# FFT and two-layer MLP kernel: half of the turns as quarter products, filters in places of their own, second slot's first product ahead of V's second half

## The reference, cut to what matters

```python
def _attn_ref(x, filt_r, filt_i):            # x: (2, 3008, 256)
    X = np.fft.rfft(x, axis=1)
    F = (filt_r + 1j * filt_i)[None, :, :]
    y = np.fft.irfft(X * F, n=x.shape[1], axis=1)
    return y.astype(np.float32)

def _moe_ref(x, w_in, w_out):                # (6016, 256) x (256, 2048) x (2048, 256)
    h = x @ w_in
    g = np.maximum(0.01 * h, h)
    return (g @ w_out).astype(np.float32)

def _moe2_ref(x, w_in, w_out):               # the same with g = relu(h) ** 2
    ...

def reference(**kwargs):
    x = _attn_ref(...).reshape(B * S, D)
    return _moe2_ref(_moe_ref(x, ...), ...)
```

## Time and profile before

| | us |
|---|---|
| median of 3 runs | 1065.01 |
| the profiled execution, its own time | 1064.64 |
| its span in the trace | 1062.5 |
| TensorE busy | 1057.0 (99% of the span) |
| VectorE (DVE) busy | 827.9 (78%) |
| ScalarE (ACT) busy | 563.3 (53%) |
| GpSimd (POOL) busy | 316.1 (30%) |

### The profile page before, as it was taken

The page is one execution under the profiler, slowest core; times in us unless marked ns, Lnnn a source line. Parts: engine busy times, 40 slices in busy tenths (PEclk is TensorE's granted clock), DMA queues, the critical chain, the costliest instruction groups (busy, mean ns, idle before and its releaser), DMA issues.

```text
span 1062.5 us, 13988 instructions
## 1 busy us (share of the span) xinstructions
PE 1057.0 (99%) x5120; PEld 879.8 (83%) x5120; DVE 827.9 (78%) x1142; ACT 563.3 (53%) x979; POOL 316.1 (30%) x287
## 2 busy tenths in 40 slices
PE   9999999999999999999999999999999999999998
PEld 9558888888888888888999888888888888888998
DVE  2877898887887887787887886887887887786666
ACT  3667564564554654555554554644554554454543
POOL 1995654434343343341321211220220220210000
PEclk9999999999999999999999999999999999999999
DMA  9696000121112112112344000100100100100100
GB/s 316 176 304 231 10 1 17 36 52 46 51 49 49 52 47 51 52 33 55 118 152 147 21 1 1 40 1 1 40 1 1 40 1 1 40 1 1 40 1 35
DMA packets 66724, 61.45 MB, mean 58 GB/s; under 512 B 40688, under 2 KB 53856, under 8 KB 66656
## 3 DMA queue, kind: packets, MB, share of 16 engines
q1 hardware_dynamic: 66160, 60.06, 18.2%
q10 hardware_dynamic: 496, 0.49, 0.1%
HBM read 36.55 MB, written 23.99 MB: 57 GB/s over the span
## 4 chain that ended last, share of the span: by engine, by line
PE 98%; DMA 1%; SPq 0%; DVE 0%; ACT 0%; issue 0%; ACTq 0%
PE PS L1046 16%; PE PS L1047 16%; PE PS L1048 16%; PE PS L1054 14%; PE PS L1055 14%; PE PS L1056 14%; PE PS L935 2%; PE PS L959 2%; PE PS L1002 1%; PE PS L1022 1%; PE PS L979 1%; DMA X<-in_x 0%; DMA zu<-U 0%; DMA V<-zu 0%; SPq L219 0%; PE PS L999 0%
## 5 line engine op out<-in xcount | busy, mean ns | idle before, releaser
L683 ACT ACTIVATE GH<-GF 128x512 fp32r<-128x512 f32 (+1 forms) x384 | 238.7, 622 | 295.3 <-DVE GF L878 154.4
L884 DVE TENSOR_TENSOR GL<-GF,GH 128x512 fp32r<-128x512 f32 (+1 forms) x384 | 273.7, 715 | 110.4 <-ACT GH L683 103.7
L1048 PE MATMUL PS<-GH,WOL 128*128 128x512 f32 (+1 forms) x768 | 295.8, 385 | 0.0
L1047 PE MATMUL PS<-GL,WOH 128*128 128x512 f32 (+1 forms) x768 | 295.8, 385 | 0.0
L1046 PE MATMUL PS<-GH,WOH 128*128 128x512 f32 (+1 forms) x768 | 295.8, 385 | 0.0
L1054 PE MATMUL PS<-XH,WIH 128*128 128x512 f32 (+1 forms) x672 | 259.5, 386 | 0.0
L1056 PE MATMUL PS<-XH,WIL 128*128 128x512 f32 (+1 forms) x672 | 258.8, 385 | 0.0
L876 DVE SCALAR_TENSOR_TENSOR GF<-GF 128x512 f32<-128x512 f32 (+1 forms) x192 | 167.5, 913 | 1.6
L1048 PEld LDWEIGHTS PS<-GH,WOL 128*128 128x128 f32 x768 | 144.2, 188 | 27.0
L1046 PEld LDWEIGHTS PS<-GH,WOH 128*128 128x128 f32 x768 | 144.2, 188 | 26.8
L1047 PEld LDWEIGHTS PS<-GL,WOH 128*128 128x128 f32 x768 | 144.2, 188 | 26.6
(11 more groups left out here) (85 smaller groups left out, 941.9 us busy)
## 6 DMA issues: line engine op xcount, KB each, us to landing
V<-zu SPq DMA_DIRECT2D x12, 512.0 KB, 5.9
zu<-U SPq DMA_DIRECT2D x31, 192.0 KB, 3.7
out_y<-YT SPq DMA_DIRECT2D x5, 1024.0 KB, 4.3
X<-in_x SPq DMA_DIRECT2D x8, 512.0 KB, 8.9
FL<-in_filt SPq DMA_DIRECT2D x16, 224.0 KB, 5.0
wi<-PWH SPq DMA_DIRECT2D x16, 224.0 KB, 2.5
wi<-PWL SPq DMA_DIRECT2D x16, 224.0 KB, 3.1
WIH<-wi SPq DMA_DIRECT2D x8, 448.0 KB, 3.4
```

What stands on the lines that cost most here:

```text
L683: nc.scalar.activation(GH[:, g, 0:width(s)], GF[:, g, 0:width(s)], ACT.Copy).then_inc(g_hi[kind], 1)
L884: nc.vector.tensor_tensor(GL[:, g, 0:w], GF[:, g, 0:w], GH[:, g, 0:w].bitcast(f32), ALU.subtract).then_inc(g_lo[kind], 1)
L1047: nc.tensor.matmul(acc, wh, xl, start=False, stop=False)
L1048: return nc.tensor.matmul(acc, wl, xh, start=False, stop=last)
```

## The change

It has five parts, all in the first 100 us or so of the program.

1. Even units are turned in another way (`turn`, `turned`): not eight transposes over the whole array, but 32 products with a 64 x 64 identity, each in one quarter of the array (64 rows, 48 columns, 64 wide). Both halves of the channels go to different banks, ACT copies each bank to every other group of 64 columns of S2, and begins when all 32 products are done. The second wait of turn, for single copies, becomes one for both copies of the unit before.
2. In the loop turn(i+3) now stands ahead of spectrum(i+2).
3. Each filter has a place of its own (FLA, FLB), so no load waits for a product of DVE; six are loaded at once, the others after a spectrum or after a store.
4. POOL's sums and splits of chunks 1 and 2 leave the loop and are done behind it, with those of the other chunks; the roundings of chunks 1 and 2 on DVE move to behind the loop too, and two of ACT's go to slots 1 and 2 of the MLP.
5. up_1(1) is made right behind up_1(0), ahead of sequence(12), and the first piece of V's second half is loaded in two parts, with a semaphore of its own for the first (`v_first`).

```diff
-    FL = at("FL", [KR, FSLOTS, 2, 2 * 128], f32, 12 * KB)
+    FLA = at("FLA", [KR, F_EARLY, 2, 2 * 128], f32, o_wi + 7 * KB)
+    FLB = at("FLB", [KR, UNITS - F_EARLY, 2, 2 * 128], f32, 12 * KB)
...
@@ SP
             def load_filter(i):
-                if i >= FSLOTS:
-                    sp.wait_ge(prod, 3 * (i - FSLOTS + 1))
-                elif i == 0:
+                if i == F_EARLY:
                     for half in range(2):
                         sp.wait_ge(n1_ps[half], CH // 2)
...
+            for n in range(3):
+                sp.wait_ge(p_ps, 4 * n + 4)
+                load_filter(6 + n)
+                if n < 2:
+                    load_w1i(3 + n)
             for i in range(UNITS):
-                if i + FSLOTS < UNITS:
-                    load_filter(i + FSLOTS)
                 store_u(i)
-                if i in (1, 2, 4, 6):
-                    load_w1i(WI_EARLY + (1, 2, 4, 6).index(i))
+                if 9 + i < UNITS:
+                    load_filter(9 + i)
+                if i in (1, 2):
+                    load_w1i(4 + i)
...
-            for g in range(MH // 4):
+            first = zu[1].rearrange("j s m e -> (j s) m e")
+            sp.dma_start(V[1][:, 0:2, :, :].rearrange("p m b d -> p m (b d)"), first[:, 0:2, :]).then_inc(v_first, 16)
+            sp.dma_start(V[1][:, 2:4, :, :].rearrange("p m b d -> p m (b d)"), first[:, 2:4, :]).then_inc(v_in[1][0], 16)
+            for g in range(1, MH // 4):
                 load_v(1, g)
@@ POOL
-            for part in range(2):
-                wi_sums(1, part)
             for i in range(UNITS):
...
-                if i in (1, 3, 6):
-                    wi_split(1, (1, 3, 6).index(i))
-                if i in (8, 11):
-                    wi_sums(2, (8, 11).index(i))
...
-            for part in range(3):
-                wi_split(WI_EARLY - 1, part)
-            for k in range(WI_EARLY, WI_SEAM):
+            for k in (1, 2, 3, 4):
                 for part in range(2):
                     wi_sums(k, part)
-            for part in range(3):
-                wi_split(WI_EARLY, part)
+            for k in (1, 2):
+                for part in range(3):
+                    wi_split(k, part)
+            for part in range(2):
+                wi_sums(5, part)
             pool.wait_ge(x0_lo, 4)
@@ ACT
             def turned(i):
-                for b in range(B):
-                    act.wait_ge(s2_ps, 2 * i + b + 1)
-                    nc.scalar.activation(S2[:, i % 2, b, :, :].rearrange("p j d -> p (j d)"), PS[0:KR, b, :], ACT.Copy).then_inc(s2_sb, 1)
+                if i % 2:
+                    ...
+                else:
+                    act.wait_ge(s2_ps, 6 * (i // 2) + 4)
+                    for h in range(2):
+                        nc.scalar.activation(S2[:, i % 2, :, :, 64 * h:64 * h + 64].rearrange("p b j d -> p (b j) d"),
+                                             PS[0:KR, h, :].rearrange("p (n d) -> p n d", d=64), ACT.Copy).then_inc(s2_sb, 1)
@@ DVE
-                if i == 0:
-                    wi_round(1)
...
-            wi_round(WI_EARLY - 1)
             back(UNITS - 2)
             dve.wait_ge(yf_sb, 2 * UNITS)
             y_copy(1)
             back(UNITS - 1)
             y_copy(5)
+            wi_round(1)
+            wi_round(2)
@@ TensorE
+                if i >= 1:
+                    pe.wait_ge(s2_sb, 2 * i)
                 for b in range(B):
-                    if i >= 1:
-                        pe.wait_ge(s2_sb, 2 * i - 1 + b)
                     for k in range(UJ):
                         q = 2 * (UJ * u + k)
+                        if i % 2:
+                            ...
+                        for h in range(2):
+                            d = slice(64 * h, 64 * h + 64)
+                            c = 64 * (UJ * b + k)
+                            for part in range(2):
+                                mm = nc.tensor.matmul(PS[IM * part:IM * part + R, h, c:c + 64], TT1[half][d, b, q + part, 0:R],
+                                                      DM[d, 2, d], start=True, stop=True)
...
             for i in range(UNITS):
+                if i + 3 < UNITS:
+                    turn(i + 3)
                 if i + 2 < UNITS:
                     spectrum(i + 2)
-                if i + 3 < UNITS:
-                    turn(i + 3)
...
             up_1(0)
+            up_1(1)
             for c in range(CH, 19):
                 sequence(c)
```

More of the change, by code:

```diff
@@ L25 @@
 RING = 6
-FSLOTS = 6
+F_EARLY = 10
 RINGS = 3
@@ L104, in fft_mlp_kernel @@
         warm_sb = sem("warm_sb")
-        ft_in = [sem(f"ft_in{g}") for g in range(FSLOTS)]
+        ft_in = [sem(f"ft_in{i}") for i in range(UNITS)]
         tw_in = sem("tw_in")
@@ L263, in _ @@
             load_w1i(1)
-            for i in range(FSLOTS):
+            for i in range(6):
                 load_filter(i)
@@ L473, in _ @@
             for part in range(3):
-                wi_split(5, part)
+                wi_split(4, part)
             wo_split(2)
-            wi_split(6, 0)
+            wi_split(5, 0)
             after_splits(3)
+            wi_split(5, 1)
+            wi_split(5, 2)
             x_forms(1, 0)
             wo_split(3)
-            wi_split(6, 1)
             after_splits(4)
@@ L484, in _ @@
             wi_sums(7, 1)
+            wi_split(6, 0)
+            after_splits(5)
+            wi_split(6, 1)
             wi_split(6, 2)
-            after_splits(5)
             wo_split(4)
             x_split(1, 0)
-            wi_split(7, 0)
             after_splits(6)
-            wi_split(7, 1)
-            wi_split(7, 2)
+            for part in range(3):
+                wi_split(7, part)
+            wo_split(5)
             x_split(1, 1)
-            wo_split(5)
             after_splits(7)
@@ L543, in turned @@
             def turned(i):
-                for b in range(B):
-                    act.wait_ge(s2_ps, 2 * i + b + 1)
-                    nc.scalar.activation(S2[:, i % 2, b, :, :].rearrange("p j d -> p (j d)"), PS[0:KR, b, :], ACT.Copy).then_inc(s2_sb, 1)
+                if i % 2:
+                    for b in range(B):
+                        act.wait_ge(s2_ps, 6 * (i // 2) + 5 + b)
+                        nc.scalar.activation(S2[:, i % 2, b, :, :].rearrange("p j d -> p (j d)"), PS[0:KR, b, :], ACT.Copy).then_inc(s2_sb, 1)
+                else:
[3 more added lines that the diff above has]
+                                             PS[0:KR, h, :].rearrange("p (n d) -> p n d", d=64), ACT.Copy).then_inc(s2_sb, 1)
             def back(i):
@@ L735, in _ @@
                     wo_round(k + 2)
[L736 to L737 removed]
+                if s in (1, 2, 4):
+                    wi_round((5, 6, 7)[s // 2])
                 late = 1 if p == 0 else 0
@@ L923, in _ @@
             pe.wait_ge(warm_sb, 1)
-            for _ in range(8):
-                nc.tensor.matmul(PS[:, 0, 0:128], WARM[:, :], WARM[:, :], start=True, stop=True)
+            for h in range(2):
+                for k in range(UJ):
+                    nc.tensor.matmul(PS[:, h, 128 * k:128 * k + 128], WARM[:, :], WARM[:, :], start=True, stop=True)
             pe.wait_ge(dft_in, 16)
@@ L953, in turn @@
                     pe.wait_ge(n1_late, 2)
+                if i == 1:
+                    pe.wait_ge(n1_pad, 2)
+                if i >= 1:
+                    pe.wait_ge(s2_sb, 2 * i)
                 for b in range(B):
-                    if i >= 1:
-                        pe.wait_ge(s2_sb, 2 * i - 1 + b)
                     for k in range(UJ):
                         q = 2 * (UJ * u + k)
-                        mm = nc.tensor.transpose(PS[0:KR, b, 128 * k:128 * k + 128],
-                                                 TT1[half][:, b, q:q + 2, :].rearrange("p q r -> p (q r)")[:, 0:KR], DM[:, 2, :])
-                    mm.then_inc(s2_ps, 1)
+                        if i % 2:
+                            mm = nc.tensor.transpose(PS[0:KR, b, 128 * k:128 * k + 128],
+                                                     TT1[half][:, b, q:q + 2, :].rearrange("p q r -> p (q r)")[:, 0:KR], DM[:, 2, :])
+                            if k == UJ - 1:
+                                mm.then_inc(s2_ps, 1)
+                            continue
+                        for h in range(2):
+                            d = slice(64 * h, 64 * h + 64)
+                            c = 64 * (UJ * b + k)
+                            for part in range(2):
+                                mm = nc.tensor.matmul(PS[IM * part:IM * part + R, h, c:c + 64], TT1[half][d, b, q + part, 0:R],
+                                                      DM[d, 2, d], start=True, stop=True)
+                                if b == B - 1 and k == UJ - 1:
+                                    mm.then_inc(s2_ps, 1)
             def spectrum(i):
@@ L1007, in sequence @@
                 half, g, b = c // CH, c % CH // 2, c % 2
-                pe.wait_ge(v_in[half][g], 16)
```

(8 more changed lines are left out.)

21 lines of the change are left out of this document (10 added, 11 removed).

## The result

The changed kernel takes 1067.88 us (median of 22 runs, 1066.06 to 1068.76), the kernel before 1065.08 (22 runs, 1064.23 to 1068.3). The ratio is 1.0021 [1.0015, 1.0027]: 0.2% slower, inside the half per cent that the prediction called no change, and inside its range, but 2.0 us above its number and outside the 1065 to 1066.8 to which it gave 0.6. The profiled execution of the changed kernel took 1066.31 us, with a span of 1064.1, against 1064.64 and 1062.5.

What follows compares the result with a forecast made beforehand. The prediction took TensorE's own work, busy 99% of the span, to bound the kernel. Stage -0.2 and seam +1.1 gave +0.9 on 1064.64, 1065.5 profiled and 1065.9 us for the median; range 1062.9 to 1068.5.

Steps and rivals of the forecast that it cites:

- The quarter turn: Loop of units: a quarter turn takes 0.9 us, an even unit 2.62 instead of 2.90; six units gain 1.7 us.
- New waits at the head: Start of the unit stage: spectrum(0) waits 0.3 us for ACT, turn(3) 0.45 more; 0.8 us lost in all.
- The loop's other limit: Loop: the path from spectrum over DVE to POOL's sums needs 5.5 us, so inverse waits, 0.4 us over the stage.
- The 0.3 for inverse(15): End of the unit stage: DVE does units 14 and 15 back to back, so inverse(15) waits 0.3 us.
- The seam: Before sequence(12): V's 1.2 us wait goes, up_1(1) waits 2.25 us for POOL's split of chunk 1; +1.1 us.
- the sum: Stage -0.2 and seam +1.1 make +0.9 us on the profiled 1064.64; median 0.4 above that, so 1065.9 us.
- Nor does its load in two parts: Before sequence(12): loading V in two parts doesn't matter, as sequence(12) is queued behind up_1(1).
- The rest: Filters and MLP: filters bring nothing, ACT's two roundings cost nothing, following products are tighter by at most 0.7 us.
- the seam's debt is passed on: Rival: group_d(0) and first down products come 0.7 us closer to DVE's and ACT's work, plus roundings; +1 to +2, chance 0.12.
- the median of the runs is 0.4 above it: Last step: the median of the changed kernel's runs lies 0.4 us above its profiled execution, 1065.9 against 1065.5.

Runs made afterwards that it cites:

- E6: The changed kernel with all its turns made by transposes; 1067.64 us, ratio to before 1.0018.
- E11: E8 with all turns as quarter products; 1067.49 us, ratio to before 1.0018.
- E12: E9 with the turn first in its unit, all turns by transposes, one wait of turn for both copies; 1065.55 us, ratio to before 1.0001.
- E10: E9 with the change's turns (quarter products in even units, turn first in its unit), filters and POOL's order as before; 1065.72 us, ratio 1.0000.
- E2: The changed kernel with POOL's splits of chunk 1 ahead of chunk 4's sums, and ACT's rounding of chunk 4 later; 1066.91 us, ratio to before 1.0017.
- E7: The changed kernel with the edits of E2 and E3 together; 1065.72 us, ratio to before 1.0000.
- E9: The kernel before with up_1(1) right behind up_1(0) and nothing else, V undivided; 1065.15 us, ratio to before 0.9993.
- E3: The changed kernel with POOL's sums of chunk 6 moved right behind chunk 5's; 1066.72 us, ratio to before 1.0009.
- E8: E7 with V's second half loaded in whole pieces as before the change; 1065.24 us, ratio to before 0.9996.
- E4: The changed kernel with eight useless products (sixteen passes) between up_1(0) and up_1(1), in the wait for POOL; 1066.52 us, ratio to before 1.0011.
- E1: The changed kernel with up_1(1) back in its old place, behind up_5(0); 1067.49 us, ratio to before 1.0016.
- E5: The kernel before with up_1(1) right behind up_1(0) and V's first piece loaded in two halves, nothing else; 1067.02 us, ratio to before 1.0014.

## Why the prediction came out as it did

**The quarter turn** was right: 0.90 us (0.9 forecast), units of 2.62 and 2.90, and six of them with the other limit bring 1.28 (1.7 - 0.4 = 1.3 forecast). 64 passes in 0.90 us start 14 ns apart on average. The rule of the Trainium skill that the prediction weighed ("TensorE: Matmul & The Clock Gate", "Wait — 56ns, not 53.3ns?") would have made it 1.6, an estimate; the measurement decides against it for passes spread over the four quarters.

**New waits at the head** were right: 0.95 against 0.8 (E6 beside the changed kernel). Turn(1) comes 0.52 later behind turn(0) than in E6 and turn(3) 0.54 later behind turn(2), though the timeline shows only 0.19 of each as idle time, where the forecast had a wait of 0.45 ahead of turn(3).

**The loop's other limit** was right in place and size: 5.60 a pair, and 5.51 where TensorE has less to do (E11). The 0.3 for inverse(15) did not come; the new order gave 0.2 (53.48 in E6, 53.68 before), which the prediction didn't have, and only with POOL's chunk work and the filters moved: without that it cost 0.6 (E12). So the stage gained 0.4 to 0.5 instead of 0.2.

**The seam** was right to a tenth: chunk 1 ready at 87.34 (87.3 forecast), a wait of 2.20, +1.13 (+1.1 forecast). Its terms were right too: the four sets took 9.02 us (75.95 to 84.97; 8.9 forecast), 1.40 of it by DVE's two roundings and two operations beside them (1.26 forecast). It is not independent of the stage, as the sum has it: POOL's chunk work is what the loop was freed of. Left in the loop (E10), it costs the new turns up to 1.3 us there (54.49 against 53.16, the filters being another difference), and moved behind it, 1.1 at up_1(1). "Nor does its load in two parts" holds only while POOL is later than V: E2 and E7 took POOL's wait away, and the halves then cost 1.5 to 1.8 us.

**The step that failed** is in "The rest": "what DVE and ACT owe the following products is not tighter by more than the 0.7 us". +0.93 followed. The 0.7 alone was not the trouble (17.11 us in E9 against 17.98): most of the loss came with POOL's moved work, likely by chunk 6's sums, which had come to lie beside DVE's three operations of 0.95 instead of 0.68 (E3, E8). The prediction had priced such collisions for POOL at the seam, and none for DVE behind it. It is what the rival "the seam's debt is passed on" priced at +1 to +2, with a chance of 0.12, but by roundings on ACT and the 0.7 us; ACT's two roundings cost nothing (behind the first down product both kernels are alike). The prediction argued against it that TensorE waited nowhere behind 86.77 before, which says nothing of how much room was left there.

**The other step that failed** is the last of the sum, "the median of the runs is 0.4 above it". It took the offset of the kernel before for the changed one. The 2.2 us wait lets the granted clock fall in about half of the runs, and their median is 1.9 us later (1068.37 against 1066.51): the median stands 1.6 above the profiled execution. E4 shows this cause. So the sum would be 1064.64 - 0.41 + 1.13 + 0.93 = 1066.3 for an execution at full clock, as measured, and 1.6 more for the median. That the median came out near the 1067.5 of the rival "passed on" is luck: less than half of the 2.0 us above the forecast is of its kind.

**What the change could bring.** Each of its gains ended in a wait: the quarter turns in the head, the early up_1(1) in POOL, the divided V in the second piece. Behind these stands the next, DVE in the MLP's head, slowed by POOL's sums wherever they were put (E8). With POOL's two delays out and V undivided (E8) it stands level with before, and the simplest part, up_1(1) early by itself (E9), is as good. Neither is told from the kernel before.

## What to carry to other kernels

When a transfer is split so that its first part lands sooner, work out the next piece too: it is now needed earlier and lands later. When work of an engine off the path is moved out of a busy stage, list for each later stage what then lies beside it, for a wait (POOL at up_1(1)) and for operations that slow each other (sums beside DVE). A wait on TensorE costs more than its length if the clock falls behind it, so compare medians of runs, not one profile. And compare the gaps of two profiles only at the same clock: an execution that lost some time to a lower clock hides the gaps behind it (E2, E3).

## What the runs showed of the hardware

- TensorE's granted clock fell from 2.4 to 1.2 GHz behind a standstill of 2.2 us in about half of the runs (12 of 22, 7 of 11, 5 of 12), behind 1.8 to 1.9 us in 13 of 35 (E1, E2, E5), behind 1.0 to 1.5 us in 8 of 125 (before beside E1 to E12, E7, E9). It came back within the next 4 us of work (0.57, then 1.00). Useless products in the wait nearly ended it (1 of 11, E4). E11's four runs and E10's one don't fit this list, as no wait in their profiles is that long.
- Passes of 64 columns in the four quarters of the array ran 14 ns apart on average.
- A change between whole-array and quarter products costs 0.16 us here too (1.02 against 0.86).
- DVE's operations on two inputs of 512 columns took 0.92 to 0.95 instead of 0.68 beside POOL's sums (changed, E2, E8), and POOL's sums up to 0.90 instead of 0.46 in the seam, where DVE worked too.
- Two loads of 256 KB landed 3.1 us after their issue, but the five of 512 KB behind them took 7.9 us (median), where six whole ones took 6.1.
- With 64 instead of 8 records of products in every turn, TensorE stood still twice, for 0.92 and 0.61 us, with no releaser in the trace (E11).
